# RWKV attention in front of two dense layers: 32-token score blocks on 64x32 tiles, updated in place, two chunks in step

## What is computed

```python
for t in range(S):
    cur = u * k[t] (outer) v[t]
    y[t] = r[t] @ (state + cur)
    state = w[t][:, None] * state + k[t] (outer) v[t]
x = y as (B, S, 384)
x = x + relu(layernorm(x) * g @ w_ch1) @ w_ch2
h = relu(x @ w_in); u, v = halves of h
v = w_spatial @ normalised(v) + b_spatial
out = (u * v) @ w_out
```

## Time and profile before

| | |
|---|---|
| median of 3 runs | 480.67 us (480.61 to 480.84) |
| profiled execution, its own time | 481.9 us |
| its span, first to last instruction | 480.1 us |
| mean granted TensorE clock | 0.982 |
| PE busy, share of the span | 436.2 us, 91% |
| DVE, ACT, POOL busy | 244.6, 234.0, 139.2 us |
| first instruction of the attention on PE | 7.46 us |
| first product of the dense layers | 182.32 us |

### The profile page before, as it was taken

One profiled execution on the slowest core, in us unless ns is written; L12 is line 12 of the kernel. 1 busy time (PEld: TensorE's weight loads), 2 busy tenths in 40 slices (PEclk: granted clock), 3 DMA queues, 4 the chain that ended last, 5 costly groups with the idle time before them and its releaser, 6 DMA issues.

```text
span 480.1 us, 7972 instructions
## 1 busy us (share of the span) xinstructions
PE 436.2 (91%) x2724; PEld 415.4 (87%) x2724; DVE 244.6 (51%) x564; ACT 234.0 (49%) x570; POOL 139.2 (29%) x198
## 2 busy tenths in 40 slices
PE   3688777877888889999999999999999999999997
PEld 3588777866777879999999999999999998899997
DVE  6887889886777863125432431334241674403120
ACT  4888898888898883322222322332221752211111
POOL 6475765656656672500000000100010530000000
PEclk9979999998899989999999999999999999999999
DMA  7424343243332121200000000000500110010102
GB/s 205 153 72 123 96 122 86 72 125 101 115 111 72 34 59 35 66 1 1 1 0 1 2 0 1 0 1 0 194 5 1 33 34 2 0 51 0 51 2 96
DMA packets 26539, 25.49 MB, mean 53 GB/s; under 512 B 1666, under 2 KB 21890, under 8 KB 26500
## 3 DMA queue, kind: packets, MB, share of 16 engines
q1 hardware_dynamic: 26500, 24.99, 18.0%
HBM read 22.62 MB, written 2.36 MB: 52 GB/s over the span
## 4 chain that ended last, share of the span: by engine, by line
PE 77%; issue 9%; DVE 7%; ACT 5%; DMA 1%; SPq 0%; DVEq 0%; ACTq 0%
PE bank L1150 20%; PE bank L1152 19%; PE bank L1151 19%; PE bank L1055 11%; ACT rz L586 2%; DVE score L802 2%; PE bank L1128 2%; DVE rin L781 1%; ACT score L642 1%; PE bank L1099 1%; PE bank L1112 1%; PE bank L1098 1%; PE bank L1235 1%; DVE wtot L762 1%; DMA kin<-in_kT 1%
## 5 line engine op out<-in xcount | busy, mean ns | idle before, releaser
L1055 PE MATMUL bank<-rz,k 128*128 128x128 f32 x576 | 86.9, 298 | 32.2 <-issue 24.6
L1055 PEld LDWEIGHTS bank<-rz,k 128*128 128x128 f32 x576 | 76.3, 206 | 40.2 <-issue 33.0
L586 ACT COPY rz<-rin 64x256 f32<-64x256 f32 x144 | 58.4, 405 | 19.6 <-DVE rin L781 18.2
L524 POOL TENSOR_TENSOR vrstd<-vmv,half 128x1 f32<-128x1 f32 x12 | 7.7, 642 | 156.6 <-DVE vmv L1001 156.6
L802 DVE COPY_PREDICATED score<-msk,bank 128x512 f32<-128x512 int32 x48 | 50.1, 1044 | 0.6
L781 DVE TENSOR_TENSOR rin<-rin,wtot 128x256 f32<-128x256 f32 x60 | 27.3, 455 | 33.5 <-ACT rz L586 32.7
L507 POOL TENSOR_TENSOR k<-k,wtot 128x256 f32<-128x256 f32 x60 | 43.0, 717 | 3.8 <-ACT k L611 1.3
L690 ACT ACTIVATE h10h<-bank 128x384 fp32r<-128x384 f32 x24 | 11.8, 490 | 50.1 <-PE bank L1152 50.1
L918 DVE SCALAR_TENSOR_TENSOR h11l<-bank,h11h 128x384 fp32r<-128x384 f32 x24 | 13.4, 558 | 37.7 <-ACT h11h L690 37.7
L918 DVE SCALAR_TENSOR_TENSOR h10l<-bank,h10h 128x384 fp32r<-128x384 f32 x24 | 13.4, 558 | 35.7 <-ACT h10h L690 35.7
L611 ACT COPY k<-k 128x256 f32<-128x256 f32 x72 | 29.5, 410 | 2.4 <-POOL k L505 0.6
(11 more groups left out here) (159 smaller groups left out, 1177.7 us busy)
## 6 DMA issues: line engine op xcount, KB each, us to landing
stage<-in_w SPq DMA_DIRECT2D x12, 384.0 KB, 3.2
vin<-in_v SPq DMA_DIRECT2D x12, 288.0 KB, 2.9
rin<-in_rT SPq DMA_DIRECT2D x12, 256.0 KB, 4.6
win<-in_wT SPq DMA_DIRECT2D x12, 256.0 KB, 3.7
kin<-in_kT SPq DMA_DIRECT2D x12, 256.0 KB, 4.3
out<-ob SPq DMA_DIRECT2D x12, 192.0 KB, 1.9
stage<-in_w_in SPq DMA_DIRECT2D x4, 384.0 KB, 3.2
x<-in_w_sp SPq DMA_DIRECT2D x4, 384.0 KB, 4.7
```

Of the source, the lines that this page charges most:

```text
L586: last = sc.copy(dst, src[lo:hi, :, :, :])
L1055: mm = te.matmul(b_level[n % 3][:, a * P:(a + 1) * P], kk[:, a, :], rz[l][:, a, :, :].rearrange("p e t -> p (e t)"), start=True, stop=True)
```

## The change

Each chunk keeps one r and one k tile. `k_left` and `r_right` multiply in place, and each must therefore wait until the level's matmuls have read the tile. `pad`, `k_right`, `k_pairs` and `with_u` are gone, with `rz`, `kc` and `k1u`. The matmuls read each head's r and k directly, so their contraction is over 64 partitions. Levels 1 to 16 (five of them) work in blocks of 32 tokens: for each pair of heads, each of four blocks and each of two heads a matmul with a stationary operand of 64 x 32 and 16 moving columns, 32 matmuls a level (`near_level`). The own term is 32 more, with 32 columns (`own_term`, with `uk` made by ACT from k and u). Levels 32 and 64 are 16 matmuls each, of 32 and 64 columns (`far_level`). Matmuls that follow each other take turns among eight such tiles of the array: two halves of its rows (the two heads) by four groups of 32 columns (the four blocks).

The levels' results are 128 x 8 x 16. DVE selects five of them and the own term into `near` (128 x 8 x 32), ACT places `near` in `score` in four copies. The low levels have one pair of banks, and the high ones have one.

Chunks go in 13 steps of 4 slots: in slot j of step s, level j of chunk s stands next to level 4 + j of chunk s - 1 (slot 3 has no high level). `turn_k` and `attend` of chunk s - 1 close the step. `gain` stands in the next step's slot 0. `decays` handles two chunks in one instruction, except for chunks 0 and 1. v comes without gaps, the state is kept as 128 x 4 x 48 and widened by ACT (`widen`). The DMA of k, r and u for chunk 0 goes ahead of that of w.

```diff
-        kin = [place(f"kin{q}", [P, NPR, P]) for q in range(3)]
-        kc = {c: place(f"k_{c}", [P, NPR, P]) for c in LEVELS[1:] + [P]}
-        rz = [place(f"rz{l}", [P, NPR, 2, P // 2]) for l in range(NL)]
-        score = [place(f"score{q}", [P, H, P]) for q in range(2)]
+        kin = [place(f"kin{q}", [P, NPR, P]) for q in range(4)]
+        win = [place(f"win{q}", [P, 2 * NPR, P]) for q in range(2)]
+        uk = place("uk", [P, NPR, P])
+        near = [place(f"near{q}", [P, H, Q]) for q in range(2)]
+        score = place("score", [P, H, P])
...

             def k_left(i, n):
...
+                level_done(pool, i, n)
+                k = halves(kin[i % 4][:, :, :], c)[0]
+                wr = run_ends(wt(i, c), 1)
...
+                    last = gp.tensor_tensor(k, k, wr[:, :, :, None].to_broadcast([P, NPR, m, c]), ALU.mult)
...

+            def near_level(i, n):
+                c = LEVELS[n]
+                if n:
+                    r_ready(te, i, n - 1)
+                    k_ready(te, i, n - 1)
+                if 1 <= n < N_LOW:
+                    te.wait_ge(low_placed, N_LOW * i + n)
+                elif n == N_LOW and i:
+                    te.wait_ge(blocks_placed, 2 * i)
+                dst = low if n < N_LOW else high
+                for a in range(NPR):
+                    for s0 in range(0, P, Q):
+                        for e, (lo, hi) in enumerate(HALF):
+                            r = rin[i % 4][lo:hi, a, s0:s0 + Q].rearrange("p (m two c) -> p m two c", two=2, c=c)
+                            mm = te.matmul(dst[s0:s0 + Q, NPR * e + a, 0:Q // 2], kin[i % 4][lo:hi, a, s0:s0 + Q],
+                                           r[:, :, 1, :], start=True, stop=True)
+                mm.then_inc(low_done if n < N_LOW else high_done, 1)
...
+            for s in range(NT + 1):
+                for j in range(N_LOW):
+                    if s < NT:
+                        if j == 0:
+                            own_term(s)
+                        near_level(s, j)
+                    if s >= 1 and j == 0:
+                        near_level(s - 1, N_LOW)
+                    elif s >= 1 and j < N_HIGH:
+                        far_level(s - 1, N_LOW + j)
+                    if j == 0 and s >= 2 and carries(s - 2):
+                        gain(s - 2)
+                    if j == 2 and 3 <= s < 3 + TG:
+                        turn(s - 3, "XT", 0, s - 3)
+                    if j == 3 and s >= 1:
+                        if carries(s - 1):
+                            turn_k(s - 1)
+                        if s < NT:
+                            attend(s - 1)
```

More of the change, by code:

```diff
@@ L48, in rwkv_moe_kernel @@
     NT = B * CH
-    VP = 3 * HD
     KC = D // P
@@ L853, in x_stats @@
+                if first(i):
+                    ve.tensor_copy(state[:, :, :], src).then_inc(state_ready, 1)
+                else:
+                    ve.tensor_tensor(state[:, :, :], sdec[:, :, :], src, ALU.add).then_inc(state_ready, 1)
             def x_stats(i, part):
@@ new lines, in _ @@
+            decays(0, 0)
+            for s in range(NT + 1):
+                for j in range(N_LOW):
+                    if s < NT:
+                        r_right(s, j)
+                    if s >= 1 and j < N_HIGH:
+                        r_right(s - 1, N_LOW + j)
+                    if j == 0 and s < NT:
+                        own_select(s)
+                    if s < NT:
+                        select(s, j)
+                    if j == 0 and s >= 1:
+                        select(s - 1, N_LOW)
+                    for i, n in decay_plan(s, j):
+                        decays(i, n)
+                    if j == 0:
+                        if 3 <= s < 3 + TG:
+                            norm(s - 3)
+                        if s >= 2 and carries(s - 2) and not first(s - 2):
+                            decay_state(s - 2)
+                    if j == 1 and s >= 2 and carries(s - 2):
+                        next_state(s - 2)
+                    if j == 2 and s >= 2:
+                        for part in range(3):
+                            x_stats(s - 2, part)
+                    if j == 3 and 3 <= s < 3 + TG:
+                        turned_lo(s - 3, "XT", 0, s - 3)
@@ L965, in _ @@
             for n in range(EARLY):
                 h1_lo(n)
-            for i in (NT - 2, NT - 1):
-                for part in range(3):
-                    x_stats(i, part)
+            for part in range(3):
+                x_stats(NT - 1, part)
             tr, vu = TG, 0
@@ new lines, in far_level @@
+            def far_level(i, n):
+                c = LEVELS[n]
+                r_ready(te, i, n - 1)
+                k_ready(te, i, n - 1)
+                if n == N_LOW + 1:
+                    te.wait_ge(middle_placed, i + 1)
+                else:
+                    te.wait_ge(blocks_placed, 2 * i + 1)
+                for a in range(NPR):
+                    for t0 in range(c, P, 2 * c):
+                        for s0 in range(t0 - c, t0, Q):
+                            for e, (lo, hi) in enumerate(HALF):
+                                mm = te.matmul(high[s0:s0 + Q, NPR * e + a, 0:c], kin[i % 4][lo:hi, a, s0:s0 + Q],
+                                               rin[i % 4][lo:hi, a, t0:t0 + c], start=True, stop=True)
+                mm.then_inc(high_done, 1)
@@ L1116, in turn, with gain @@
+            def gain(i):
+                te.wait_ge(kt_ready, carried(i))
+                for a in range(NPR):
+                    for e, (lo, hi) in enumerate(HALF):
+                        mm = te.matmul(b_turn[lo:hi, a * HD:(a + 1) * HD], kt[:, a, lo:hi], vin[i % 3][:, 2 * a + e, :],
+                                       start=True, stop=True)
+                mm.then_inc(gain_done, 1)
             def turn(t, step, g, a):
@@ L1123, in turn @@
                     src = x[:, i, :]
+                if step == "XT" and g == 0:
+                    te.wait_ge(state_ready, carried(i + 1))
                 if t and b_tr(step, g, a) is b_turn:
@@ L1172, in _ @@
                 first_product(0, f)
-            for a in range(NPR):
-                attend(NT - 1, a)
+            attend(NT - 1)
             tr, vu = TG, 0
```

703 lines of the change are left out of this document (301 added, 402 removed).

## The result

| | before | after |
|---|---|---|
| median of 4 runs, us | 480.75 (480.61 to 482.24) | 543.68 (542.59 to 544.52) |
| ratio after/before, 95% interval | | 1.130 (1.127 to 1.133) |
| profiled execution, us (span) | 481.9 (480.1) | 543.22 (541.4) |
| first product of the dense layers, us | 182.32 | 242.56 |
| from there to the end, us | 297.8 | 298.9 |

The kernel became 63 us slower (13%). The first product comes 60.2 us later, and what follows it takes 1.1 us more than in the earlier trace rows: nearly all of the time was lost in the attention.

The account below looks back on a forecast made before the run. PE was taken as the bound, though in the attention four engines run in step, none full. 7.6 + 16.2 + 251.1 + 7.4 = 282.3 us to the first dense product against 182.3: +100.0, so 581 us, range 465 to 725.

Parts of the forecast that it names:

- the main case: Attention's small matmuls: loads one by one at the full clock, 0.0315 us a pair, 581 us; chance 0.33.
- the last rival: Attention at the lower clock, L and attend doubled; with tiles side by side a step of 18.7, 528 us; chance 0.12.
- the prediction's own sum: Start, step 0, eleven steps and last step up to the first dense product; a pair at 0.012 us gives 471 us.
- Where the time changes: Only the attention before the dense layers' first product changes; the stretch behind it stays 298 us.
- The price of a small pair, 0.0315 us: Load of 32 columns and its pass on PE: 0.005 + 32 x 0.00083 us, between 0.012 and 0.111.
- 550 us by my sum: Attention's small matmuls: about 60 cycles overhead each, some 0.025 us a pass, if loads hid beside it.
- Slots: Four slots of an attention step, each with PE's levels and exposed DVE work: 8.1, 4.4, 5.2 and 5.1 us.
- tiles side by side at the full clock: Rival for the attention's small matmuls: different tiles overlap, L 0.77 us, a step 13.7, 471 us; chance 0.27.
- A step: The four attention slots together: 22.8 us, eleven times, 251.1 us; break-even at about 14.6 us.
- All lie beside PE in this forecast: ACT, DVE, POOL and DMA edits, halved decay instructions included, run beside PE and were costed at nothing.
- The select in each slot's path: One pair of low-level banks makes PE wait for select (L807), about 1.1 us a slot, 1.8 in slot 0.
- ACT's and POOL's edits at nothing: Attention: ACT loses pad and k_right, gains copies and activations; POOL loses with_u; no time counted for either.

Follow-up runs that it names:

- same_tile: Changed kernel with the low levels' and own term's matmuls reordered so the four of one tile stand together: 606.22 us, 62.5 more.
- fill: Changed kernel plus five 128-column matmuls on the identity behind each of slots 0 to 2, results thrown away: 545.58 us, 1.9 more.
- q64: Changed kernel with low levels and own term in blocks of 64 tokens on 64x64 tiles, 120 score matmuls a chunk instead of 224: 540.61 us.
- q64_all: Changed kernel with 64-token blocks, w loaded early, select first, and four identity matmuls behind each of slots 0 to 2: 486.20 us, 1.011 of before.

## Why the prediction was right, and where it was not

Sign and range were right (581 predicted, 465 to 725, 543.7 measured), the mechanism of the main case was not, and part of it was luck. The likeliest case had a full clock and pairs one by one; what came was tiles side by side at the lower clock, the last rival, 528 us at a chance of 0.12. With the pairs as measured and nothing else changed, the prediction's own sum says 471 us, faster. So the sign came out right by things that the main case did not have: the low clock, and some 40 us of waits that no sum had. That 581 lies near is luck, since a price nearly three times too high stood in for both.

- **Where the time changes**: only before the first product. Right: 298.9 us behind it against 297.8.
- **The price of a small pair, 0.0315 us ("if loads go one after another")**: this step failed. Pairs follow each other every 0.010 to 0.012 us, though the clock is the lower one. `same_tile` shows the other side: 0.030 us on one tile after another, and 62.5 us more. The argument "loads in the trace never overlap" came from loads that all fill the array, and says nothing of smaller ones. I also held against it that a matmul's two pairs use one tile; that did not make a pair cost 0.03. The Trainium skill's rule in "TensorE: Matmul & The Clock Gate", Part 3, that matmuls on different tiles run at once, was the right one: in the level at 107.68 the passes start 4 to 6 and 11 to 13 ns apart in turn where nothing disturbs them, against its 4 ns. The Trainium skill's rule in "TensorEngine Tiling (Array Packing)", section Instruction Overhead, some 60 cycles for each matmul and 550 us by my sum, was near in time for a wrong reason: with the tiles in turn no pair costs 0.025 us on tiles of 32 columns.
- **Slots** (8.1, 4.4, 5.2, 5.1 predicted; with tiles side by side at the full clock 4.4, 2.9, 2.6, 3.9): the step shown takes 4.0, 3.3, 2.9 and 9.8. The first three are near the side-by-side case, with a stop of 0.6 us in the second. The last is its 3.9, plus 2.9 for 28 pairs of 128 columns at 0.213 instead of 0.111, plus the wait of 2.93 for L859: 9.7.
- **A step**: 22.8 predicted, 18.7 by the rival. Steps 1 to 10 take 16.5 to 26.8 us, 20.1 on average. The side-by-side step of 13.7 and 2.9 for the clock make 16.6, and the three shortest steps take 16.5, 17.1 and 17.3.
- **The rival's own sum**: it says that L and attend double, but by that its step would be some 22 us and its time some 560. Its 18.7 comes out with L = 1.1 us, for which no row stood; the level shown took 0.73. `attend` and `turn_k` did double.
- **The clock**: the likeliest case took the full one. It was 1.2 GHz through the attention, and `turn_k` and `attend` are 2.8 us a step slower by it (`fill`), 31 us over eleven steps, an estimate. In the 64-token version the full clock in part of the attention is worth 23.2 us, fillers paid.
- **"The DMAs are as many … All lie beside PE in this forecast"**: failed. Two transfers are not hidden: w, that the paired decays ask for one chunk sooner, and PE's own program. The sum counted the instructions' time on the engine and not their way to it.
- **"halves the decays' instructions"** was costed at nothing; the pairing makes DVE wait 26.6 us in 4 waits. Three of them lie mostly beside `turn_k` and `attend`. Taking them away is worth 10.8 us with half of the matmuls and 2.3 in the full kernel, where the stops for instructions grow by 5.9.
- **`turn_k` behind a turned tile (L859)**: 13.8 us in 3 waits, not in the sum. They share a bank, `b_turn`. The longest, 8.8 us, is DVE's wait for w seen from PE: with w early the three come to 7.7, the longest 2.9. No run took the rest away.
- **The select in each slot's path**: right in kind, PE waits for L807 for 0.8 to 1.5 us in the step shown and 1.2 on average (35.4 us, 29 times), 1.1 predicted. Putting it first gave 8.4 us, until POOL and the instructions became the bound.
- **ACT's and POOL's edits at nothing**: nearly so. Neither is a releaser of PE's main waits in the changed kernel (2.5 us for POOL's L500, 1.7 for ACT's L605). But it is POOL's splitting of the weights that SP's queue waits for ahead of w, and once the select stands first, `k_left` is next in line with 12.7 us.

Where the 63 us come from, as an estimate: 471 us for side by side at the full clock, 31 to 32 for the clock, and the remaining 41 for the waits for w, for L859 and for instructions. These overlap each other, so their sums (26.6, 13.8, 34.5 us) can't be added. Open stay their split on and off the path, and whether a version with 32-token blocks, a full clock and enough instructions would beat the kernel before.

## What to carry to other kernels

Before a full-size matmul is cut into small ones, count three things apart: how often neighbours use the same tile (0.030 against 0.0115 us a pair here, both at 1.2 GHz), how many instructions a microsecond the new stream takes, and what the idle time between the small groups does to the clock under the large matmuls that stay. When two parts that used to run chunk by chunk are paired, look at the issue order of the second one's input. Ask of a wait beside what it lies before pricing it: of DVE's 26.6 us only some 10 held PE. And what one wait gives back another can take: the same edit was worth 2.3 us with the stops for instructions there and 10.8 without them.

## What the runs showed of the hardware that I had not expected

- **PE can outrun the supply of its program.** With two instructions every 0.010 us it stops 126 or 127 pairs apart or a multiple, until 1.2 to 1.6 us behind the end of a 16 KB packet: 26 stops, 0.35 to 3.9 us long. With pairs 0.030 apart 2 stops were left, with half of the pairs 3, with 64 x 64 tiles none. Why some stops are ten times as long as others is not shown.
- **Pairs on tiles of 32 columns hardly follow the clock**: a level of 64 takes 0.60 us from first load to last at 1.2 GHz (changed kernel) and 0.53 at 2.4 (`fill`), medians. On tiles of 64 columns they do: 32 pairs take 0.75 us (`q64`) and 0.44 (`q64_all`).
- **Where the record of the clock is missing, the clock was low.** The page printed 1.00 for an attention in which loads of 128 columns were 0.21 us apart; a near twin of the kernel had 0.53 on record at the same spacing. In every trace here that has a record, it begins with a 1.00. The kernel before shows what stands ahead of it: its record begins at 12.4 us, and its loads are 0.213 us apart until then and 0.112 from there.

```profile
7.43 1.78 PEld L1055 LDWEIGHTS bank<-rz,k1u 128*128 128x128 f32 x8 [7.43 <-issue]
13.60 0.97 PEld L1055 LDWEIGHTS bank<-rz,k 128*128 128x128 f32 x8 [0.62 <-issue]
```

The spacing of known instructions is the surer reading.
